# Retention ahead of two MLPs: the batches' chunks alternate, and scores and state use four quarters of the array

## The chip, the core and the metric

The kernel runs on one core of a Trainium2 chip. Its engines work side by side, each through its own instructions in order: PE (TensorE, with PEld for its weight loads), ACT (ScalarE), DVE (VectorE), POOL (GpSimd) and SP (SyncE), which issues nearly all transfers. They wait for one another by semaphores. The metric is the time of one execution on the device, in microseconds.

## The reference

```python
# q, k, v: batch 2, 8 heads, 576 positions, 64 features
scores = scale * np.matmul(q, k.transpose(0, 1, 3, 2))
Dmat = np.where(rel >= 0, gamma[:, None, None] ** rel[None, :, :], 0.0)   # rel = i - j
attn = np.matmul(scores * Dmat, v)
x = attn.transpose(0, 2, 1, 3).reshape(B * S, H * D)                      # 1152 x 512
for e in range(4):                                                        # F = 1024
    out += p[:, e:e + 1] * (np.maximum(x @ w1[e], 0.0) @ w2[e])
h = out @ w_in                                                            # 2048 wide
g = h * np.tanh(softplus(h))
return g @ w_out
```

## The kernel before

**Retention.** The sequence of a batch is cut into 9 chunks of 64 positions, 18 in all (`CHUNKS`). Inside a chunk the masked scores of 64 queries and 64 keys times v are taken; what comes from earlier chunks is a state, k transposed times v for each head. A decay factor for each key is put into v ahead (`v_decay`, POOL) and one for each query into the output (`decayed`, DVE), so the mask is of zeros and ones and the state is a plain sum, which stays in PSUM. A chunk is one transfer of 512 KB into one of six slots of `qkv`: partitions 0 to 63 (`KEYS`) hold v and k by positions, 64 to 127 (`FEATS`) hold k and q by features. An output is one matmul of 128 rows for each head: the masked scores (which replace k in `KEYS`, `masked` on DVE) and q (in `FEATS`) against v (`KEYS`) and the state, which ACT copies out of PSUM over k of the next chunk (`state_copy`). Batch 0's nine chunks come first, then batch 1's. All matmuls of the retention are fp32; each shows as two records in the trace.

**Turns.** 19 turns (`TURNS`) run on PE. Turn c has the scores of chunk c+1 and the state of chunk c, interleaved by heads (`scores_and_state`, lines 448 and 452), then the output of chunk c-1 (`output`, line 488). Scores read rows 64 to 127 of the array and write 64 columns, state reads rows 0 to 63 and writes the other 64. Between them stand halves of tiles of layer one of expert 0 (`AFTER_SCORES`, `AFTER_OUTPUT`): a tile is 128 of the 1024 hidden features for the first 384 tokens (`plain_products`), four inner blocks of three fp32r matmuls (`three`, lines 494 to 496: high by high, high by low, low by high), and needs the first six chunks' x. Eight tiles fit in turns 7 to 18. `keep_warm` runs matmuls on zeros (line 626): 9 ahead of chunk 0, 5 behind its scores, 3 in turn 0 and 8 in turn 6.

**The other engines in a turn.** DVE: `masked`, `decayed` of the chunk before, at times `rows` (a table of decay), `plain_lo` (the low half of a relu tile, line 849), `first_lo` (the low half of x, line 843). ACT: `state_copy` (line 696), `plain_hi` (relu and high half, line 713), `first_hi` (line 702), `job_hi` for weights (line 368; sums: line 364). POOL: `v_decay` two chunks ahead (line 1025), `job_lo` (line 395; a job of kind "s" makes four sums of weight blocks, lines 382 to 387, and their low half, line 390). `IN_TURN` says which weight jobs stand in which turn, one for each; the eight raw slots of weights (`RAW`) come free as jobs finish.

**Behind the turns** PE runs layer two of the first four tiles (`second(0, q)`, q = 0 to 11, three for each of w2's first four units), then stages of seven products by sums of blocks (`product`; the first that needs sums of x is P6) with layer two of the stage before between them, for four experts and the last MLP. DVE and ACT make the sums of x once the last chunk is through.

**Transfers.** SP loads chunk 0, the table of decays and mask, then chunks 1 to 5, then by turns a weight unit (256 KB) and a chunk, from weight 0 behind the landing of chunk 3. ACT loads the probabilities and the rest of the table.

## Time and profile before

| what | value |
|---|---|
| median of 3 runs | 626.67 us (625.93 to 629.63) |
| profiled execution, first to last instruction | 625.2 us |
| PE busy | 618.1 us (99%) |
| DVE, ACT, POOL busy | 271.6, 237.0, 285.0 us (43%, 38%, 46%) |
| chain that ended last | PE 97% |
| granted clock of TensorE | 1.00 |
| loaded from HBM | 47.45 MB, 80 GB/s over the span |

Busy is the share of the span in which an engine had an instruction running. PE's share counts pipelined matmuls and the filler on zeros alike. In the timelines each line gives the start in us from the first instruction, the time taken, the engine, the line of the kernel, the operation, what it writes and reads, its shape and the count where like ones were merged; in brackets the idle time of the engine ahead of it and what ended it. "issue" is an end that the profile does not show.

### The profile page before, as it was taken

To read this page: it belongs to the slowest core of one execution; us is meant where nothing else is said; L and a number is where in the kernel's file an instruction comes from. 1 tells how busy PE (TensorE), PEld (TensorE's weight loads), DVE (VectorE), ACT (ScalarE), POOL (GpSimd) and SP (SyncE) were. 2 spreads that over 40 slices of the span, in tenths; PEclk is the share of its full clock that TensorE was granted. 3 is DMA by queue.
4 is the path that set the end of the run, shared out by engine and by line. 5 is a ranking of instruction groups with operands and counts; after the bars stand their busy time and mean duration, and the time that the engine had idled before them with its cause. 6 is when DMAs were issued, how large, how long until landed. Compare 5 with 4: busy or idle time off the path is not lost.

```text
span 625.2 us, 9507 instructions
## 1 busy us (share of the span) xinstructions
PE 618.1 (99%) x3773; PEld 553.7 (89%) x3773; DVE 271.6 (43%) x388; ACT 237.0 (38%) x459; POOL 285.0 (46%) x239
## 2 busy tenths in 40 slices
PE   8999999999999999999999999999999999999997
PEld 5788899999999999999999899988989999989996
DVE  5646854433154433154433154434545432324334
ACT  3446423432223432123442223435455454334431
POOL 4657645553435542535543635532435553443300
PEclk9999999999999999999999999999999999999999
DMA  8955312332102321212312212321211233201002
GB/s 271 318 185 174 106 48 68 101 89 63 51 35 68 102 79 57 68 35 67 102 67 69 69 35 67 88 81 35 68 34 35 68 117 85 68 0 52 1 0 102
DMA packets 25147, 50.43 MB, mean 81 GB/s; under 512 B 2896, under 2 KB 3216, under 8 KB 25104
## 3 DMA queue, kind: packets, MB, share of 16 engines
q1 hardware_dynamic: 24816, 49.66, 25.4%
q8 instruction: 31, 0.51, 0.3%
q10 hardware_dynamic: 288, 0.17, 0.1%
q14 instruction: 12, 0.10, 0.0%
HBM read 47.45 MB, written 2.36 MB: 80 GB/s over the span
## 4 chain that ended last, share of the span: by engine, by line
PE 97%; DMA 1%; DVE 1%; issue 0%; ACT 0%; SPq 0%; DVEq 0%; ACTq 0%
PE bank L494 31%; PE bank L496 30%; PE bank L495 30%; PE bank L448 2%; PE bank L488 2%; DMA qkv<-in_chunks 1%; PE bank L619 1%; PE bank L452 1%; PE bank L626 0%; DVE acc_sb L895 0%; DVE acc_sb L899 0%; ACT qkv L696 0%; DVE qkv L822 0%; DVE h_lo L856 0%; SPq L418 0%
## 5 line engine op out<-in xcount | busy, mean ns | idle before, releaser
L395 POOL TENSOR_TENSOR w_lo<-w_raw,w_hi 128x512 fp32r<-128x512 f32 x96 | 132.2, 1389 | 150.7 <-ACT w_hi L368 148.9
L494 PE MATMUL bank<-w_hi,h_hi 128*128 128x512 f32 x432 | 168.8, 391 | 0.0
L496 PE MATMUL bank<-w_hi,h_lo 128*128 128x512 f32 x432 | 168.4, 390 | 0.0
L495 PE MATMUL bank<-w_lo,h_hi 128*128 128x512 f32 x432 | 168.3, 390 | 0.0
L882 DVE TENSOR_TENSOR h_act<-part,bank 128x384 f32<-128x384 f32 x96 | 52.9, 552 | 169.7 <-PE bank L496 168.9
L390 POOL TENSOR_TENSOR ws<-ws_f,ws 128x1024 fp32r<-128x1024 f32 x24 | 57.6, 2400 | 145.1 <-ACT ws L364 145.1
L496 PEld LDWEIGHTS bank<-w_hi,h_lo 128*128 128x128 f32 x432 | 81.1, 188 | 16.9
L495 PEld LDWEIGHTS bank<-w_lo,h_hi 128*128 128x128 f32 x432 | 81.1, 188 | 12.3
L494 PEld LDWEIGHTS bank<-w_hi,h_hi 128*128 128x128 f32 x432 | 81.0, 188 | 12.2
L732 ACT ACTIVATE part<-bank 128x384 f32<-128x384 f32 x72 | 35.4, 491 | 139.3 <-PE bank L496 139.3
L849 DVE SCALAR_TENSOR_TENSOR h_lo<-h_act,h_hi 128x384 fp32r<-128x384 f32 x64 | 74.3, 1170 | 20.6 <-ACT h_hi L722 20.0
L494 PE MATMUL bank<-xa_hi,w_hi 128*128 128x384 f32 x192 | 66.4, 346 | 0.0
L496 PE MATMUL bank<-xa_hi,w_lo 128*128 128x384 f32 x192 | 64.5, 336 | 0.0
L495 PE MATMUL bank<-xa_lo,w_hi 128*128 128x384 f32 x192 | 64.4, 336 | 0.0
L856 DVE TENSOR_TENSOR h_lo<-h_act,h_hi 128x384 fp32r<-128x384 f32 x48 | 38.2, 797 | 55.5 <-ACT h_hi L727 55.1
L368 ACT ACTIVATE w_hi<-w_raw 128x512 fp32r<-128x512 f32 x96 | 57.2, 618 | 0.0
L722 ACT ACTIVATE h_hi<-h_act 128x384 fp32r<-128x384 f32 x64 | 33.5, 525 | 58.5 <-DVE h_act L882 58.5
L495 PE MATMUL bank<-xt,ws 128*128 128x384 f32 x144 | 48.4, 336 | 0.0
L496 PE MATMUL bank<-xt,ws 128*128 128x384 f32 x144 | 48.4, 336 | 0.0
L494 PE MATMUL bank<-xt,ws 128*128 128x384 f32 x144 | 48.4, 336 | 0.0
L849 DVE SCALAR_TENSOR_TENSOR h_lo<-bank,h_hi 128x384 fp32r<-128x384 f32 x32 | 17.7, 554 | 59.9 <-ACT h_hi L713 59.9
L713 ACT ACTIVATE h_hi<-bank 128x384 fp32r<-128x384 f32 x32 | 15.7, 491 | 73.7 <-PE bank L496 73.7
(87 smaller groups left out, 911.4 us busy)
## 6 DMA issues: line engine op xcount, KB each, us to landing
w_raw<-in_weights SPq DMA_DIRECT2D x144, 256.0 KB, 2.8
qkv<-in_chunks SPq DMA_DIRECT2D x18, 512.0 KB, 4.6
out<-acc_sb SPq DMA_DIRECT2D x6, 256.0 KB, 2.0
out<-acc_sb SPq DMA_DIRECT2D x1, 768.0 KB, 3.6
consts<-in_consts ACTq DMA_DIRECT2D x1, 146.0 KB, 3.6
ident<-in_consts SPq DMA_DIRECT2D x1, 64.0 KB, 4.0
consts<-in_consts SPq DMA_DIRECT2D x1, 34.0 KB, 3.9
p_nat<-in_probs ACTq DMA_DIRECT2D x1, 18.0 KB, 3.6
```

The costliest lines, as they stand in the source:

```text
L368: act.activation(w_hi[int(kind == "w2")][:, x], w_raw[:, r % RAW], ACT.Copy).then_inc(s_wh, 1)
L390: pool.tensor_tensor(w_sum(x)[:, 1], ws_f[:, :], w_sum(x)[:, 0].bitcast(F32), ALU.subtract)\
L395: pool.tensor_tensor(w_lo[layer][:, x], w_raw[:, r % RAW], w_hi[layer][:, x].bitcast(F32), ALU.subtract).then_inc(s_wl, 1)
L494: pe.matmul(out, w[0], x[0], start=first, stop=False, **more)
L495: pe.matmul(out, w[0], x[1], start=False, stop=False, **more)
L496: return pe.matmul(out, w[1], x[0], start=False, stop=last, **more)
L713: act.activation(h_hi[:, tile_slot(s, i)], banks[6 + i % 2][:, 0:TC], ACT.Relu).then_inc(s_hh, 1)
L722: act.activation(h_hi[:, tile_slot(s, i)], h_act[:, i % 2], ACT.Relu).then_inc(s_hh, 1)
L732: act.activation(part[:, i], banks[6][:, 0:TC], ACT.Copy).then_inc(s_pt, 1)
L849: dve.scalar_tensor_tensor(h_lo[:, slot], full, 0.0, h_hi[:, slot].bitcast(F32), ALU.max, ALU.subtract).then_inc(s_hl, 1)
L856: dve.tensor_tensor(h_lo[:, slot], h_act[:, i % 2], h_hi[:, slot].bitcast(F32), ALU.subtract)\
L882: dve.tensor_tensor(h_act[:, i % 2], part[:, kept], banks[bank][:, 0:TC], op).then_inc(s_cc, 1)
```

## The change

- The chunks of the two batches alternate: chunk c is number c // 2 of batch c % 2 (`place`, `batch`). Each batch has a PSUM bank for its state. Tokens come out in this order, and the host puts them back.
- Decayed values go to a ring of four tiles `sv` (rows `KEYS`); the state for chunk c+2 is copied into its `FEATS` rows. v and k in the slot are no longer overwritten by them. POOL and ACT wait for the output that last read the place of the ring.
- Heads with even and odd number write the scores to the lower and the upper 64 partitions, likewise the state: scores of two heads and state of two heads follow each other on the four quarters of the array. The mask is two instructions of DVE, one for each half of the partitions.
- Outputs of the first six chunks alternate between banks 6 and 3.
- Tiles stand whole behind the output, in turns 7, 8, 10, 11, 13, 14, 16, 17. Relu and its low half stand first in the next turn on ACT and DVE. `first_lo` is one turn later, but for chunk 5. Weight jobs are moved (`JOBS_IN`): w2's first three units stand earlier, the sum job in turn 17, w2's units 3 to 5 in turn 18.
- The table and chunk 0 are one transfer on SP. Weights start behind the landing of chunk 6, ahead of chunk 8, one unit with each chunk.
- The filler is 7 and 3 matmuls; none in the turns.

```diff
...
+SLOT = 2 * HEADS * CH
+RING = 4
+def batch(c):
+    return c % BATCH
+def place(c):
+    return c // BATCH
 def has_state(c):
-    return c % PER_BATCH < PER_BATCH - 1
+    return place(c) < PER_BATCH - 1
...
-AFTER_SCORES = {8: (0, 1), 9: (1, 1), 10: (2, 1), 11: (3, 1), 12: (4, 1), 13: (5, 0), 14: (5, 1),
-                15: (6, 0), 16: (6, 1), 17: (7, 0), 18: (7, 1)}
-AFTER_OUTPUT = {7: (0, 0), 8: (1, 0), 9: (2, 0), 10: (3, 0), 11: (4, 0)}
-HIDDEN_IN = {t: c for c, (t, half) in AFTER_SCORES.items() if half}
-ROWS_IN = {0: 4, 1: 5, 6: 6, 7: 7, 8: 8}
-WARM_IN = {0: 3, 6: 8}
+TILE_IN = {7: 0, 8: 1, 10: 2, 11: 3, 13: 4, 14: 5, 16: 6, 17: 7}
+JOBS_IN = {6: (("w1", 0, 0),), 7: (("w1", 0, 1),), 8: (("w1", 0, 2),), 9: (("w1", 0, 3),), 10: (("w2", 0, 0),),
+           11: (("w1", 0, 4),), 12: (("w1", 0, 5),), 13: (("w2", 0, 1),), 14: (("w1", 0, 6),), 15: (("w1", 0, 7),),
+           16: (("w2", 0, 2),), 17: (("s", 0, 0),), 18: (("w2", 0, 3), ("w2", 0, 4), ("w2", 0, 5))}
+ROWS_IN = {5: 4, 9: 5, 11: 6, 13: 7, 15: 8}
+WARM_START, WARM_NEXT = 7, 3
...
+        sv = sb("sv", [P, RING, HEADS, DH])
...
-        ps_o = banks[3][:, 0:PAIRS * CH].rearrange("p (h c) -> p h c", h=PAIRS)
+        by_pairs = [bank[:, 0:PAIRS * CH].rearrange("p (h c) -> p h c", h=PAIRS) for bank in banks]
+        ps_s, ps_state = by_pairs[0:SCORES], by_pairs[4:4 + BATCH]
...
+        def ps_o(c):
+            return by_pairs[6 if c < PER_BLOCK and c % 2 == 0 else 3]
+        def score_rows(x):
+            return (KEYS, FEATS)[x]
+        def state_rows(x):
+            return (FEATS, KEYS)[x]
...
-            load_chunk(0)
-            sp.dma_start(consts[KEYS, 0:ROW0], consts_in[KEYS, 0:ROW0]).then_inc(s_const, 16)
+            sp.dma_start(loaded[:, lead - CONSTS:lead + SLOT], first_in).then_inc(s_slot[0], 16)
             load_chunk(1)
-            for c in range(2, 6):
-                if c > 2:
-                    chunk_there(c - 3)
-                load_chunk(c)
-            for u in range(UNITS):
-                chunk_there(3 + u)
-                load_weights(u)
-                chunk_there(4 + u)
-                load_chunk(6 + u)
-            for c in range(6 + UNITS, CHUNKS):
+            load_chunk(2)
+            for c in range(3, 8):
                 chunk_there(c - 3)
                 load_chunk(c)
-                load_weights(UNITS + c - 6 - UNITS)
-            sp.dma_start(ident[:, :], consts_in[:, CONSTS:]).then_inc(s_id, 16)
-            for r in range(UNITS + CHUNKS - 6 - UNITS, len(LOADS)):
+            for c in range(8, CHUNKS):
+                chunk_there(c - 2)
+                load_weights(c - 8)
+                load_chunk(c)
+            sp.dma_start(ident[:, :], ident_in).then_inc(s_id, 16)
+            for r in range(CHUNKS - 8, len(LOADS)):
                 load_weights(r)
...
-                return pe.matmul(ps_s[c % SCORES][:, h], by_feats(c, 0)[:, h], by_feats(c, 1)[:, h],
+                return pe.matmul(ps_s[c % SCORES][score_rows(h % 2), h // 2], by_feats(c, 0)[:, h], by_feats(c, 1)[:, h],
                                  start=True, stop=True)
             def state_head(c, h):
-                return pe.matmul(ps_state[h // HS][:, h % HS], by_keys(c, 1)[:, h], by_keys(c, 0)[:, h],
-                                 start=(c % PER_BATCH == 0 and h % HS == 0), stop=True, skip_group_check=True)
+                return pe.matmul(ps_state[batch(c)][state_rows(h % 2), h // 2], by_keys(c, 1)[:, h], sv[KEYS, c % RING, h],
+                                 start=(place(c) == 0 and h < 2), stop=True, skip_group_check=True)
...
-                        pe.wait_ge(s_sm, n - SCORES + 1)
+                        pe.wait_ge(s_sm, 2 * (n - SCORES + 1))
                 if has_state(c):
                     pe.wait_ge(s_vd, c + 1)
-                for h in range(HEADS):
-                    if has_state(c) and c > 0 and h % HS == 0:
-                        pe.wait_ge(s_st, 2 * states(c - 1) - 1 + h // HS)
+                    if place(c) > 0:
+                        pe.wait_ge(s_st, 2 * states(c - BATCH))
+                for hp in range(PAIRS):
                     if n < CHUNKS:
-                        mm = scores_head(n, h)
-                        if h == HEADS - 1:
+                        for x in range(2):
+                            mm = scores_head(n, 2 * hp + x)
+                        if hp == PAIRS - 1:
                             mm.then_inc(s_sc, 1)
                     if has_state(c):
-                        mm = state_head(c, h)
-                        if h == HEADS - 1:
+                        for x in range(2):
+                            mm = state_head(c, 2 * hp + x)
+                        if hp == PAIRS - 1:
                             mm.then_inc(s_kv, 1)
             def output(c):
                 pe.wait_ge(s_vd, c + 1)
-                pe.wait_ge(s_sm, c + 1)
+                pe.wait_ge(s_sm, 2 * (c + 1))
                 rows = KEYS
-                if c % PER_BATCH > 0:
+                if place(c) > 0:
                     rows = slice(0, P)
-                    pe.wait_ge(s_st, 2 * states(c - 1))
-                if c > 0:
+                    pe.wait_ge(s_st, 2 * states(c - BATCH))
+                if c >= PER_BLOCK:
                     pe.wait_ge(s_xt, c)
+                elif c > 1:
+                    pe.wait_ge(s_xt, c - 1)
                 for hp in range(PAIRS):
                     for x in range(2):
-                        mm = pe.matmul(ps_o[DH * x:DH * (x + 1), hp], qkv[rows, c % SLOTS, 0, 2 * hp + x],
+                        mm = pe.matmul(ps_o(c)[DH * x:DH * (x + 1), hp], sv[rows, c % RING, 2 * hp + x],
                                        qkv[rows, c % SLOTS, 1, 2 * hp + x], start=True, stop=True)
                 mm.then_inc(s_o, 1)
...
-            keep_warm(WARM)
+            keep_warm(WARM_START)
             pe.wait_ge(s_slot[0], landed(0))
             for h in range(HEADS):
                 mm = scores_head(0, h)
             mm.then_inc(s_sc, 1)
-            keep_warm(5)
+            keep_warm(WARM_NEXT)
             for c in range(TURNS):
                 if c < CHUNKS:
                     scores_and_state(c)
-                if c in AFTER_SCORES:
-                    plain_half(*AFTER_SCORES[c])
-                keep_warm(WARM_IN.get(c, 0))
                 if c > 0:
                     output(c - 1)
-                if c in AFTER_OUTPUT:
-                    plain_half(*AFTER_OUTPUT[c])
+                if c in TILE_IN:
+                    s, i = divmod(TILE_IN[c], ITEMS)
+                    plain_ready(s, i)
+                    plain_products(s, i, range(KT))
...
             def state_copy(c):
-                act.wait_ge(s_sc, c + 2)
                 act.wait_ge(s_kv, states(c))
-                for i in range(2):
-                    at = by_feats(c + 1, 0)[:, HS * i:HS * (i + 1)]
-                    act.activation(at, ps_state[i], ACT.Copy).then_inc(s_st, 1)
+                if c >= BATCH:
+                    act.wait_ge(s_o, c - BATCH + 1)
+                for x in range(2):
+                    act.activation(sv[FEATS, (c + BATCH) % RING, x::2], ps_state[batch(c)][state_rows(x)],
+                                   ACT.Copy).then_inc(s_st, 1)
...
             for c in range(TURNS):
+                if c - 1 in TILE_IN:
+                    plain_hi(*divmod(TILE_IN[c - 1], ITEMS))
                 if c < CHUNKS and has_state(c):
                     state_copy(c)
-                for t, at in HIDDEN_IN.items():
-                    if at == c:
-                        plain_hi(t // ITEMS, t % ITEMS)
...
-                dve.tensor_tensor(by_keys(c, 1), ps_s[c % SCORES], mask.unsqueeze(1).broadcast_to([CH, HEADS, CH]),
-                                  ALU.mult).then_inc(s_sm, 1)
+                for x in range(2):
+                    at = score_rows(x)
+                    dve.tensor_tensor(by_keys(c, 1)[:, x::2], ps_s[c % SCORES][at],
+                                      mask[at].unsqueeze(1).broadcast_to([CH, PAIRS, CH]), ALU.mult).then_inc(s_sm, 1)
...
             for c in range(TURNS):
+                if c - 1 in TILE_IN:
+                    plain_lo(*divmod(TILE_IN[c - 1], ITEMS))
                 if c < CHUNKS:
                     masked(c)
+                if c > 1 and c != PER_BLOCK + 1:
+                    first_lo(c - 2)
                 if c > 0:
                     decayed(c - 1)
                 if c in ROWS_IN:
                     rows(ROWS_IN[c])
-                for t, at in HIDDEN_IN.items():
-                    if at == c:
-                        plain_lo(t // ITEMS, t % ITEMS)
-                if c > 0:
+                if c == PER_BLOCK:
                     first_lo(c - 1)
+            first_lo(CHUNKS - 1)
...
             def v_decay(c):
                 pool.wait_ge(s_slot[c % SLOTS], landed(c))
-                v = by_keys(c, 0)
-                pool.tensor_tensor(v, v, key_decay[KEYS, c % PER_BATCH].unsqueeze(2).broadcast_to([CH, HEADS, DH]),
+                if c >= RING:
+                    pool.wait_ge(s_o, c - RING + 1)
+                pool.tensor_tensor(sv[KEYS, c % RING], by_keys(c, 0),
+                                   key_decay[KEYS, place(c)].unsqueeze(2).broadcast_to([CH, HEADS, DH]),
                                    ALU.mult).then_inc(s_vd, 1)
...
-                    pool.wait_ge(s_xl, c)
+                    if c > 1:
+                        pool.wait_ge(s_xl, c - 1)
                     job_lo(pool, job)
...
+        "first": np.concatenate([tables(), chunks[0].reshape(P, SLOT)], axis=1),
+        "chunks": chunks[1:],
+        "ident": np.eye(P, dtype=np.float32),
+        "probs": moe_domain_probs.reshape(BATCH, PER_BATCH, CH, MOE_EXPERTS).transpose(0, 2, 1, 3).reshape(P, -1),
         "weights": np.concatenate(weights),
...
-    nc = bacc.Bacc("TRN2", target_bir_lowering=False, num_devices=1)
+    nc = bacc.Bacc("TRN2", target_bir_lowering=False, num_devices=1, dynamic_dma_scratch_size=1024)
...
+    rows = run(nc, [{f"in_{n}": a for n, a in arrays.items()}], core_ids=[0]).results[0]["out"]
+    return np.ascontiguousarray(rows.reshape(PER_BATCH, BATCH, CH, DM).transpose(1, 0, 2, 3).reshape(TOKENS, DM))
```

## Rows read from the trace of the kernel before

**Rows 1.** Busy time by stretch: us, engine busy (instructions), clock, DMA share, GB/s.

```profile
0.00:62.20 62.20, 58.49 (x954) 46.59 (x954) 35.44 (x71) 29.32 (x72) 37.59 (x39) 1.00 0.71 238
62.20:625.20 563.00, 559.59 (x2824) 507.07 (x2820) 236.16 (x318) 207.69 (x389) 247.44 (x201) 1.00 0.21 63
```

**Rows 2.** Timeline of PE: start us, us, engine, line, operation, out<-in.

```profile
1.31 3.64 PE L626 MATMUL bank<-zeros 128*128 128x512 bf16 x9 [1.31 <-POOL zeros L1019]
5.95 1.25 PE L626 MATMUL bank<-zeros 128*128 128x512 bf16 x5
...
31.22 0.27 PE L448 MATMUL bank<-qkv 64*64 64x64 f32 x1
32.30 0.45 PE L494 MATMUL bank<-xa_hi,w_hi 128*128 128x384 f32 x1
...
33.54 0.69 PE L488 MATMUL bank<-qkv 128*64 128x64 f32 x16
34.16 0.44 PE L494 MATMUL bank<-xa_hi,w_hi 128*128 128x384 f32 x1
...
70.50 0.34 PE L494 MATMUL bank<-xb_hi,w_hi 128*128 128x384 f32 x1
...
72.61 0.39 PE L494 MATMUL bank<-w_hi,h_hi 128*128 128x512 f32 x1
```

**Rows 3.** Timeline of PE around 10.5 us, one line a record.

```profile
10.49 0.22 PE L448 MATMUL bank<-qkv 64*64 64x64 f32 x1
10.49 0.22 PE L488 MATMUL bank<-qkv 64*64 64x64 f32 x1
10.50 0.22 PE L452 MATMUL bank<-qkv 64*64 64x64 f32 x1
10.55 0.22 PE L452 MATMUL bank<-qkv 64*64 64x64 f32 x1
```

**Rows 4.** Busy time by stretch, the first 20 us.

```profile
0.00:12.00 12.00, 9.91 (x132) 5.91 (x134) 5.02 (x12) 2.62 (x6) 4.88 (x9) 1.00 0.80 266
12.00:16.00 4.00, 3.50 (x94) 2.97 (x89) 3.37 (x7) 2.10 (x6) 2.14 (x2) 1.00 0.91 291
16.00:20.00 4.00, 3.95 (x111) 3.59 (x113) 2.92 (x7) 2.22 (x7) 2.35 (x2) 1.00 0.94 329
```

**Rows 5.** Timeline of POOL, values of chunk 5 decayed as it landed.

```profile
13.55 1.03 POOL L1025 TENSOR_TENSOR qkv<-qkv,consts 64x512 f32<-64x512 f32 x1 [0.39 <-DMA qkv<-in_chunks]
```

**Rows 6.** Groups by line, 26 to 62 us: count, busy us, mean ns, idle before.

```profile
L843 DVE TENSOR_TENSOR xb_lo<-xf,xb_hi 128x256 fp32r<-128x256 f32 x6 | 3.4, 562 | 0.1
L837 DVE TENSOR_TENSOR xf<-bank,row_decay 128x256 f32<-128x256 f32 x10 | 4.2, 421 | 8.4 <-PE bank L488 8.4
L849 DVE SCALAR_TENSOR_TENSOR h_lo<-bank,h_hi 128x384 fp32r<-128x384 f32 x7 | 3.8, 547 | 0.0
...
L713 ACT ACTIVATE h_hi<-bank 128x384 fp32r<-128x384 f32 x7 | 3.4, 490 | 4.7 <-PE bank L496 4.7
L364 ACT ACTIVATE ws<-ws_f 128x1024 fp32r<-128x1024 f32 x1 | 1.1, 1058 | 0.5 <-POOL ws_f L387 0.5
...
L395 POOL TENSOR_TENSOR w_lo<-w_raw,w_hi 128x512 fp32r<-128x512 f32 x10 | 12.9, 1289 | 11.3 <-ACT w_hi L368 9.5 <-DVE xb_lo L843 1.8
L390 POOL TENSOR_TENSOR ws<-ws_f,ws 128x1024 fp32r<-128x1024 f32 x1 | 2.4, 2392 | 1.2 <-ACT ws L364 1.2
L382 POOL TENSOR_TENSOR ws_f<-w_raw 128x256 f32<-128x256 f32 x1 | 0.7, 747 | 0.2 <-DVE xb_lo L843 0.2
```

**Rows 7.** Line 843, x's low half: shortest, median and longest ns.

```profile
L843 DVE TENSOR_TENSOR xb_lo<-xf,xb_hi x12: 382/452/1931, 27.3 to 64.4; 128x256 fp32r<-128x256 f32 x6, 128x128 fp32r<-128x128 f32 x6
```

**Rows 8.** Timelines of PE and DVE behind 62.2 us.

```profile
62.20 0.50 PE L494 MATMUL bank<-w_hi,h_hi 128*128 128x512 f32 x1
...
74.64 0.34 PE L494 MATMUL bank<-xt,ws 128*128 128x384 f32 x1
...
70.85 0.96 DVE L925 TENSOR_TENSOR xt<-xs_a,xt 128x768 fp32r<-128x768 f32 x1
```

More of the change, by code:

```diff
@@ L135, in add @@
         JOBS.append(job)
-    for u in range(UNITS):
-        add(IN_TURN, 5 + u, "w1", 0, u)
-    for u in range(3):
-        add(IN_TURN, 12 + u, "w2", 0, u)
-    add(IN_TURN, 15, "s", 0, 0)
-    for u in range(3, 6):
-        add(IN_TURN, 13 + u, "w2", 0, u)
+    for turn, jobs in JOBS_IN.items():
+        for job in jobs:
+            add(IN_TURN, turn, *job)
     add(IN_STAGE, 1, "w2", 0, 6)
@@ L240, in build @@
         x2_c = acc_sb[:, TT:2 * TT].rearrange("p t d -> p (t d)").rearrange("p (k c) -> p k c", k=KT)
+        qkv = loaded[:, lead:].rearrange("p (s w h c) -> p s w h c", s=SLOTS, w=2, h=HEADS)
+        consts = loaded[:, lead - CONSTS:lead]
         key_decay = consts[:, 0:MASK0].rearrange("p (c h) -> p c h", h=HEADS)
[L243 removed]
+        mask = consts[:, MASK0:ROW0]
         row0 = consts[:, ROW0:STEP0].rearrange("p (h c) -> p h c", h=PAIRS)
@@ L247, in build @@
         banks = [ctx.enter_context(nc.psum_tensor(f"bank{i}", [P, 512], F32)) for i in range(8)]
-        ps_s = [banks[i][KEYS, :].rearrange("p (h c) -> p h c", h=HEADS) for i in range(SCORES)]
-        ps_state = [banks[i][FEATS, 0:HS * DH].rearrange("p (h c) -> p h c", h=HS) for i in range(2)]
-        ps_o = banks[3][:, 0:PAIRS * CH].rearrange("p (h c) -> p h c", h=PAIRS)
+        by_pairs = [bank[:, 0:PAIRS * CH].rearrange("p (h c) -> p h c", h=PAIRS) for bank in banks]
+        ps_s, ps_state = by_pairs[0:SCORES], by_pairs[4:4 + BATCH]
         s_slot = [sem(f"s_slot{i}") for i in range(SLOTS)]
-        s_const = sem("s_const")
-        s_rows = sem("s_rows")
         s_id = sem("s_id")
@@ L522, in plain_products @@
                     mm.then_inc(s_l1, 1)
-            def plain_half(t, half):
-                s, i = divmod(t, ITEMS)
-                if half == 0:
-                    plain_ready(s, i)
-                plain_products(s, i, range(2 * half, 2 * half + 2))
             def product(s, j):
@@ L830, in decayed @@
             def decayed(c):
-                i = c % PER_BATCH
+                i = place(c)
                 if i > 0:
@@ L1047, in tables @@
     c = np.arange(PER_BATCH, dtype=np.float64)
-    consts = np.zeros((P, CONSTS + P))
+    consts = np.zeros((P, CONSTS))
     keys = gamma[None, None, :] ** (MID - CH * c[None, :, None] - i[:, None, None])
     consts[KEYS, 0:MASK0] = keys.reshape(CH, MASK0)
-    consts[KEYS, MASK0:ROW0] = i[:, None] <= i[None, :]
+    consts[:, MASK0:ROW0] = np.tile(i[:, None] <= i[None, :], (2, 1))
     rows = gamma[:, None] ** (i[None, :] - MID) / np.sqrt(DH)
@@ L1088 @@
     build(nc, *args, out)
-    return run(nc, [{f"in_{n}": a for n, a in arrays.items()}], core_ids=[0]).results[0]["out"]
+    rows = run(nc, [{f"in_{n}": a for n, a in arrays.items()}], core_ids=[0]).results[0]["out"]
+    return np.ascontiguousarray(rows.reshape(PER_BATCH, BATCH, CH, DM).transpose(1, 0, 2, 3).reshape(TOKENS, DM))
```

33 lines of the change are left out of this document (12 added, 21 removed).

## The prediction

> **What bounds the kernel now.** I read the busy time by stretch first. TensorE (PE) is busy 559.6 of the 563.0 us behind 62.2 us, where the first matmul of layer two starts, and 58.5 of the 62.2 us ahead of it [rows 1]. The change leaves the work behind 62.2 us as it is (DVE, ACT and POOL are under half busy there), so its worth is how much earlier that matmul starts, minus what comes late behind it. Call its start T; T is 62.2 us now. PE hardly waits ahead of T either, but 25 matmuls of that stretch are filler on a tile of zeros (9, 5, 3 and 8 by the code), and they hide waiting.
>
> Next the timeline of PE, which gives prices from the start of one block to the start of the next [rows 2]. Scores with state: 31.22 to 32.30, 1.08 us. A half tile of layer one: 1.24 us (32.30 to 33.54). An output: 33.54 to 34.16, 0.61 us.
>
> **The four quarters.** Before, the scores use one quarter of the array and the state another: two streams of 16 records in 1.08 us. An output uses both column halves, 16 records in two streams of 8, and takes 0.61 us. With scores and state each over both column halves, 32 records run in four streams of 8, so I price the block as an output, 0.61 us, 0.47 us less. No row shows four streams. Three are there at 10.49 us: scores, output and state start within 0.01 us, and the state again at 10.55 [rows 3], 0.05 to 0.06 us later, as it does beside one other stream (1.08 us for 16 records, with 0.14 for filling and draining). The bounds are 0.61 and 1.08 us; I take 0.61, since the third stream cost nothing.
>
> The Trainium skill speaks against this: "TensorE: Matmul & The Clock Gate", section "Wait — 56ns, not 53.3ns?", says that start to start never falls below about 25 ns, however small the matmul. By that, 32 records would take 0.80 us, and an estimate by that page is a block of about 0.95 us, a saving of 0.13. The trace has starts closer than that, on different quarters, so I do not follow it.
>
> **Whole tiles.** 12 matmuls, 70.50 to 72.61 us, take 2.11 us, or 0.176 each [rows 2]. A whole tile is a half (1.24) and six more (1.04), 2.28 us, where two halves took 2.48. The change of array shape is paid once, and eight tiles save 1.6 us.
>
> **When the first tile can start.** Up to turn 7 the chunks bind. Weights no longer go ahead of chunk 8. Chunk 8 is there once 0.02 (probabilities) + 0.74 (tables and chunk 0) + 8 x 0.524 + 0.26 (the first weights) = 5.2 MB have come. The windows give 3.2 MB by 12 us, 4.4 by 16 and 5.7 by 20 [rows 4]. Chunk 5, at 3.3 MB by the same count, landed just ahead of 13.55 us [rows 5], when about 3.6 MB had come: what is in flight behind adds 0.3 to 0.4 MB. So chunk 8 lands at 5.6 MB, about 19.6 us (bounds 18.6 and 20.6: 0.3 MB more or less in flight). In turn 6 POOL decays chunk 8's values (1.03 us [rows 5]) before it makes the first weights' low half (1.29 [rows 6]), and tile 0 waits for that: 19.6 + 0.1 + 1.0 + 1.3 = 22.0 us. From turn 8 a chunk and weights, 0.79 MB, need 2.4 us, less than the 3.5 us of a turn with a tile and 2.7 on the mean of a group of three, so transfers bind no more.
>
> **From there to T, by PE alone.** 8 tiles x 2.28 = 18.2; 9 blocks of scores and state (turns 8 to 16) x 0.61 = 5.5; 11 outputs x 0.61 = 6.7. Together 30.4, so T = 52.4 us.
>
> **What is late next.** In a turn ACT now first makes the relu of the tile of the turn before, then copies state, then the high half of x, then weights; DVE makes the tile's low half, two masks, x's low half of two turns back, then the decayed output. From chunk 6 on, output c waits for the decayed output c-1. The turns behind 8, 11 and 14 have no tile, and PE runs ahead of that chain there. From the start of tile 1, PE is ready for output 9 after 2.28 + 3 x 0.61 = 4.11 us. The chain that releases it is the tile (2.40, with its drain), relu on ACT 0.49, low half 0.50, two masks 0.68, x's low half 0.36, decayed output 0.41: 4.84 us. The two masks of 64 x 256 are priced by the decayed output, which reads 256 columns of PSUM too: 0.42 each [rows 6], of which 0.08 lies under the next; x's low half is its fastest, 0.38 to 0.42, less a like overlap [rows 7]. The difference, 0.73 us, falls three times (outputs 9, 12, 15), together 2.1 us. Behind the waiting output stand tiles 2, 4 and 6, so T moves by all of it: 54.5 us.
>
> DVE's work between tiles of SBUF is slower at times: x's low half took from 0.38 to 1.93 us [rows 7], 0.56 on the mean for 128 x 256 [rows 6], and I take POOL's instructions for what holds it up. Turns are shorter now and POOL's work is the same, so I add 0.5 us to each of the three stalls, 1.5 in all (bounds 0 and 3.9, the latter where each waits for a whole POOL instruction, 1.3). T = 56.0 us.
>
> **What is late behind T.** The weight sums of job s are now in turn 17 (turn 15 before), and w2's fourth unit behind it. From T backward, tile 6 starts at T - 5.8; ACT, DVE and x's low half end 4.3 us later, at T - 1.5, and release POOL. Then four sums (4 x 0.74), the high half on ACT (1.06), the low half 2.39, the unit's low half 1.29 [rows 6]: T + 6.2. PE wants it at the tenth of twelve products, 9 x 0.69 = 6.2 us behind T (62.20 to 70.50 is 8.30 for twelve [rows 2, 8]). No margin is left. I put 0.8 us on it (bounds 0 and 1.9, with DVE's x sums between POOL's instructions). The x sums on DVE: the first low half is done at 71.8 now and wanted at 74.64 [rows 8], and DVE gets to them a little sooner relative to T, so nothing there.
>
> **At no cost.** One load in place of two and chunk 0: same bytes. Decayed values in a ring: same POOL instruction, other target. State copies: same two of ACT, now two turns ahead of use. Other host order: none. Fewer fillers: 15 gone, all ahead of tile 0, hidden behind chunk 8; without that cover they would only save.
>
> **Sum.** 62.2 - 56.0 - 0.8 = 5.4 us earlier, of 625.2: 619.8. The median shown is 626.7, 1.5 above the profiled execution, so 621.3.
>
> **Rivals.**
> A, the loop of ACT and DVE keeps up: no hindrance by POOL, no wait for w2. T = 54.5 us, gain 7.7; with chunk 8 up to a us earlier, 8.2. For it: DVE is busy 35.4 of the 62.2 us ahead of T [rows 1]. Against: the slow ones of today [rows 7]. 619.0, or 618.5. 0.32.
> B, the quarters do not overlap beyond two. The block stays at 1.08 us, nine of them cost 4.2 us more, but the three stalls (3.6 us) vanish since PE no longer runs ahead; T is 52.4 + 4.2 = 56.6, with w2's 0.8 a gain of 4.8: 621.9. For it: no row has four streams. Against: [rows 3]. 0.14. The Trainium skill's limit of 25 ns (page and section above) would land between B and my sum.
> C, the gain is given back behind T: POOL and DVE, with the same work in less time, hold w2's unit and the x sums by 2 to 4 us more. 623 to 625.5. Against: 2.8 us of margin on the x sums [rows 8]. 0.08.
> D, slower: the clock. The first nine fillers took 3.64 us, 0.40 each, the next five 1.25, 0.25 [rows 2]: PE began at half its clock (1.2 GHz) and rose to 2.4 though the page grants 1.00 all through. Seven fillers, then a wait, then 1.2 us of work per 1.6 us chunk may not lift it. At half clock a turn is 2.4 us and a tile 4.4. Every two us at half clock costs one; to be slower than before, the low level must last from tile 0 (22.0 us) for more than 11 us, to about turn 10. It would give 627 to 634, the latter if it lasts for 25 us. Against: PE is dense from tile 0, as it was here when it rose. 0.05.
>
> **Chances.** My sum 0.41 (its own range 619.5 to 622.5), A 0.32, B 0.14, C 0.08, D 0.05. About 1% (6.3 us) is what a measurement of this kernel can tell from no change: under 620.4 is faster. A but for 0.02, a quarter of my sum and 0.02 of B lie there, 0.42; slower by over 1% (from 633) is half of D, 0.03; the remainder, 0.55, is within. The range reaches over A and B and most of C: 617.5 (chunk 8 at 18.6 us and A, with half a us over) to 625.0.
>
> **What would show it.** Sixteen score and sixteen state records within 0.7 us: right for the quarters; 1.1 us: B. Tile 0 at 22.0 us. PE idle about a us ahead of outputs 9, 12 and 15, put down to DVE's decayed output. T at 56.0. A gap of PE some 6 us behind T, put down to w2's low half on POOL. Filler or score records at twice their length past 10 us: D. Wrong would be the sum if chunk 8 lands off 19.6 by a us or more, which moves T by the like, or if ACT's queue delays the relu of each tile, which my chain counts as free.

## The result, and the profile after

| | before | after |
|---|---|---|
| median | 626.81 us (625.93 to 629.63, 4 runs) | 633.48 us (631.61 to 635.27, 4 runs) |
| ratio to before, 95% interval | | 1.0104 (1.0079 to 1.0129) |
| profiled execution | 625.2 us | 633.4 us |
| T, the first matmul of layer two | 62.20 us | 66.62 us |
| from T to the end | 563.0 us | 566.8 us |
| granted clock, mean | 1.00 | 0.985 |

The change is slower by 1.0%, where 621.3 us (617.5 to 625.0) was predicted. Both halves of the program lost: T came 4.4 us later, not 6.2 earlier, and the work behind it takes 3.8 us more. The profiled execution is the slowest of the four, 1.8 us above their median and with the lowest mean clock, so what is read from it below adds up to more than the medians are apart.

From the page of the kernel after: busy time, the granted clock in 40 slices of 15.8 us, and the shares of the chain that ended last.

```profile
PE 611.6 (97%) x3758; PEld 550.4 (87%) x3758; DVE 281.9 (45%) x406; ACT 238.6 (38%) x459; POOL 288.4 (46%) x239
...
PEclk8798999999999999999999999999999999999999
...
PE 88%; DVE 8%; issue 2%; ACT 1%; DMA 1%; POOL 0%; DVEq 0%; POOLq 0%
```

PE was 97% of the chain before and is 88% now, and DVE has 8%. The granted clock, full all through before, is below full in the first slices. The busy time by stretch, cut at the new T, to be held against [rows 1]:

```profile
0.00:66.60 66.60, 51.42 (x938) 43.52 (x938) 42.63 (x88) 29.13 (x69) 34.76 (x36) 0.87 0.68 222
66.60:633.40 566.80, 560.21 (x2823) 506.90 (x2820) 239.27 (x318) 209.47 (x390) 253.66 (x204) 1.00 0.21 63
```

PE is busy 7 us less ahead of T, as the change wants, and idle 15 us there where it was idle 4. DVE is busy 42.6 us instead of 35.4.

**The quarters and the whole tile.** Timeline of PE in the kernel after: start us, us, engine, line (454 scores, 458 state, 498 output, 504 to 506 tile):

```profile
31.66 0.44 PE L504 MATMUL bank<-xa_hi,w_hi 128*128 128x384 f32 x1
...
33.94 0.27 PE L454 MATMUL bank<-loaded 64*64 64x64 f32 x2
33.96 0.27 PE L458 MATMUL bank<-sv,loaded 64*64 64x64 f32 x2
34.05 0.23 PE L454 MATMUL bank<-loaded 64*64 64x64 f32 x2
...
34.57 0.69 PE L498 MATMUL bank<-loaded,sv 128*64 128x64 f32 x16
35.18 0.27 PE L454 MATMUL bank<-loaded 64*64 64x64 f32 x2
```

The whole tile takes 2.28 us (31.66 to 33.94). The 32 records of scores and state take 0.63 us to the output's start; the output takes 0.61 more.

**The waits of PE ahead of T**, from the timeline of PE in the kernel after, the wait in brackets:

```profile
10.87 0.80 PE L498 MATMUL bank<-loaded,sv 64*64 64x64 f32 x10 [2.09 <-DVE loaded L826]
...
25.69 0.69 PE L504 MATMUL bank<-xa_hi,w_hi 128*128 128x384 f32 x1 [1.60 <-POOL w_lo L408]
...
37.18 0.69 PE L498 MATMUL bank<-loaded,sv 128*64 128x64 f32 x16 [1.30 <-DVE xf L841]
...
48.61 1.12 PE L498 MATMUL bank<-loaded,sv 128*64 128x64 f32 x16 [2.82 <-DVE xf L841]
...
59.70 0.69 PE L498 MATMUL bank<-loaded,sv 128*64 128x64 f32 x16 [1.34 <-DVE xf L841]
...
66.00 0.69 PE L498 MATMUL bank<-loaded,sv 128*64 128x64 f32 x16 [0.42 <-DVE xf L841]
```

Outputs 0, 9, 12, 15 and 17 and tile 0 stand here; a wait of 1.25 us ahead of output 6 (23.41) comes shortly before tile 0. Tile 0 starts at 25.69 us. The waits at 37.18, 48.61 and 59.70 are those of outputs 9, 12 and 15. The output at 48.61 takes 1.12 us, not 0.69.

The wait of tile 0 is put down to POOL, but it goes back to DVE. Values of chunk 8 are decayed at 21.49, as it lands; POOL is free for the first weights' low half at 22.5 us, and that starts at 24.38. The timelines of POOL and of ACT (705 x's high half, 381 weights) there:

```profile
21.49 1.03 POOL L1031 TENSOR_TENSOR sv<-loaded 64x512 f32<-64x512 f32 x1 [1.83 <-DMA loaded<-in_chunks]
24.38 1.26 POOL L408 TENSOR_TENSOR w_lo<-w_raw,w_hi 128x512 fp32r<-128x512 f32 x1 [1.85 <-ACT w_hi L381]
```

```profile
23.30 0.42 ACT L705 ACTIVATE xa_hi<-x_tmp 128x256 fp32r<-128x256 f32 x1 [1.13 <-DVE x_tmp L841]
23.62 0.61 ACT L381 ACTIVATE w_hi<-w_raw 128x512 fp32r<-128x512 f32 x1
```

ACT makes the high half of the weights only behind that of x, which had waited for a decayed output of DVE.

**The clock.** Busy time by stretch of the kernel after (the number behind the five engines is the granted clock):

```profile
10.00:15.00 5.00, 4.13 (x106) 4.05 (x108) 3.93 (x8) 1.17 (x3) 3.11 (x3) 0.58 0.71 247
15.00:25.00 10.00, 6.71 (x204) 5.68 (x200) 9.05 (x23) 6.34 (x16) 3.74 (x4) 0.84 0.85 270
25.00:30.00 5.00, 4.31 (x17) 3.87 (x21) 0.41 (x1) 1.04 (x4) 3.89 (x4) 0.50 0.86 269
```

A granted clock of 0.50 is 1.2 of 2.4 GHz. It was at 0.50 from about 10.8 to 17.5, 24.5 to 31.2 and 48.3 to 51.7 us. Tile 0 at 25.69 lasted 4.14 us, 1.86 more than a tile at full clock.

**Behind T.** The timeline of DVE in the kernel after, three of x's eight sums (lines 964 to 969 and 929):

```profile
68.69 0.95 DVE L964 TENSOR_TENSOR xs_a<-xf 128x768 f32<-128x768 f32 x1
...
70.42 3.15 DVE L967 TENSOR_TENSOR xs_a<-xf,xs_a 128x768 f32<-128x768 f32 x1
...
81.35 2.05 DVE L929 TENSOR_TENSOR xt<-xs_b,xt 128x768 fp32r<-128x768 f32 x1
```

The timeline of POOL in the same stretch, the end of a job's weight sums and then the low halves of five units:

```profile
69.67 3.09 POOL L403 TENSOR_TENSOR ws<-ws_f,ws 128x1024 fp32r<-128x1024 f32 x1 [1.24 <-ACT ws L377]
72.72 9.86 POOL L408 TENSOR_TENSOR w_lo<-w_raw,w_hi 128x512 fp32r<-128x512 f32 x5
```

And the timeline of PE, at w2's fourth unit:

```profile
74.75 0.50 PE L504 MATMUL bank<-w_hi,h_hi 128*128 128x512 f32 x1 [1.71 <-POOL w_lo L408]
```

The eight sums took 14.7 us (68.7 to 83.4), where they took 9.5 before; the fifth started at 70.85 in [rows 8] and starts at 75.55 now. A second wait of PE, 1.2 us at 84.85, is for a copy of ACT (line 735). ACT reaches it only behind the high half of a relu, which waited for DVE's addition at 83.32, and that stood behind the sums.

### The profile page after: what moved, and what is told of

Its sections match the earlier page's. It is cut to its first block, busy times and chain, and to the rows that moved or that the text cites. A ratio compares the mean times of both kernels' runs of the same rounds, so it can differ in the third digit from the quotient of the medians.

```text
span 633.4 us, 9497 instructions
## 1 busy us (share of the span) xinstructions
PE 611.6 (97%) x3758; PEld 550.4 (87%) x3758; DVE 281.9 (45%) x406; ACT 238.6 (38%) x459; POOL 288.4 (46%) x239
## 4 chain that ended last, share of the span: by engine, by line
PE 88%; DVE 8%; issue 2%; ACT 1%; DMA 1%; POOL 0%; DVEq 0%; POOLq 0%
PE bank L504 29%; PE bank L506 29%; PE bank L505 29%; DVE loaded L826 1%; DVE xt L929 1%; DVE xb_lo L847 1%; DMA p_nat<-in_probs 1%; PE bank L622 1%; DVE xf L841 1%; DVE xs_a L967 0%; ACT h_hi L716 0%; ACT w_hi L381 0%; PE bank L498 0%; DVE xa_lo L847 0%; DVE x_tmp L841 0%
## 5 line engine op out<-in xcount | busy, mean ns | idle before, releaser
L408 POOL TENSOR_TENSOR w_lo<-w_raw,w_hi 128x512 fp32r<-128x512 f32 x96 | 134.3, 1412 | 151.6 <-ACT w_hi L381 151.6
L505 PEld LDWEIGHTS bank<-w_lo,h_hi 128*128 128x128 f32 x432 | 81.1, 188 | 12.2
L735 ACT ACTIVATE part<-bank 128x384 f32<-128x384 f32 x72 | 35.4, 491 | 139.5 <-PE bank L506 139.5
```

Source lines behind the costliest of these rows:

```text
L408: pool.tensor_tensor(w_lo[layer][:, x], w_raw[:, r % RAW], w_hi[layer][:, x].bitcast(F32), ALU.subtract).then_inc(s_wl, 1)
L505: pe.matmul(out, w[0], x[1], start=False, stop=False, **more)
L735: act.activation(part[:, i], banks[6][:, 0:TC], ACT.Copy).then_inc(s_pt, 1)
```

## The experiments

The start of tile 0, T, the rest behind it and the time of x's sums come from each profiled execution, in us. Ratios are against the kernel before, on the same chip, with 95% intervals.

| kernel | tile 0 | T | rest | sums | median us | ratio |
|---|---|---|---|---|---|---|
| before | 25.79 | 62.20 | 563.0 | 9.5 | 626.8 | 1 |
| after | 25.69 | 66.62 | 566.8 | 14.7 | 633.5 | 1.0104 (1.0079 to 1.0129) |
| e1 filler in turns | 26.74 | 64.96 | 566.8 | 14.7 | 632.8 | 1.0107 (1.0084 to 1.0129) |
| e2 probabilities late | 24.09 | 64.39 | 569.8 | 14.7 | 636.1 | 1.0161 (1.0140 to 1.0182) |
| e3 decayed first | 24.90 | 60.24 | 567.0 | 15.2 | 629.4 | 1.0048 (1.0020 to 1.0077) |
| e4 two quarters | 25.48 | 61.91 | 566.5 | 14.7 | 630.0 | 1.0064 (1.0046 to 1.0081) |
| e5 e3, w2 early | 23.15 | 58.43 | 566.4 | 14.7 | 628.5 | 1.0016 (0.9995 to 1.0036) |
| e6 e3, two quarters | 26.23 | 60.98 | 566.7 | 14.7 | 628.6 | 1.0026 (1.0007 to 1.0046) |
| e7 mended | 24.66 | 58.40 | 569.2 | 14.7 | 627.2 | 0.9998 (0.9978 to 1.0017) |
| e8 e7, two quarters | 24.82 | 62.51 | 567.7 | 14.2 | 632.1 | 1.0077 (1.0055 to 1.0099) |
| e9 e7, POOL waits | 22.97 | 56.74 | 563.5 | 12.0 | 622.7 | 0.9926 (0.9907 to 0.9944) |
| e10 after, POOL waits | 24.36 | 63.14 | 565.1 | 12.5 | 630.5 | 1.0048 (1.0029 to 1.0067) |
| e11 e9, no filler in turns | 25.69 | 61.78 | 563.4 | 12.0 | 624.4 | 0.9961 (0.9944 to 0.9979) |
| e12 e9, probabilities first | 24.11 | 57.86 | 563.4 | 12.0 | 622.8 | 0.9929 (0.9906 to 0.9952) |

A single T is good to some us only: it depends on where the clock falls in that execution. After and e10 do the same up to T, and theirs are 3.5 us apart. The medians and ratios decide. Where the two differ, the ratios weigh more, since each is taken against the kernel before on the same chip.

### e1: filler that keeps the clock up

```diff
-WARM_START, WARM_NEXT = 7, 3
+WARM_START, WARM_NEXT = 9, 5
+WARM_IN = {1: 9, 6: 3, 7: 5, 10: 5, 13: 12, 16: 6}   # matmuls on zeros, ahead of a turn's output
+WARM_TILE = {7: 7}                                   # and ahead of its tile
```

> The changed kernel with matmuls on zeros where its PE waited: 9 and 5 at the start, 9 ahead of output 0, 3 ahead of output 5, 5 ahead of output 6, 7 ahead of tile 0, and 5, 12 and 6 ahead of outputs 9, 12 and 15. The changed kernel takes 633.5 us, the one before 626.8. Clock theory (PE fell to half its clock in three stretches, 10.9 to 17, 25.5 to 31 and 48 to 52 us, and that is the loss): full clock in all of them, tile 0 in 2.3 us in place of 4.1, layer two of the first tiles (66.6 us now) at 61 to 62, and 628 to 629 us. Chain theory (DVE with ACT and POOL sets the pace of the turns, and PE's clock only fills its waits): the records are short again but the waits ahead of outputs 9, 12 and 15 grow by as much, at least 631.5 us.

The clock stayed at 1.00, in its busy time by stretch:

```profile
10.00:26.70 16.70, 13.40 (x356) 9.61 (x352) 13.46 (x30) 9.50 (x25) 7.70 (x8) 1.00 0.76 274
26.70:65.00 38.30, 36.06 (x567) 29.65 (x568) 26.21 (x52) 18.08 (x44) 23.12 (x21) 1.00 0.62 202
```

The median is only 0.7 us below the kernel after, and the ratios cannot be told apart, as the chain theory had it. So lifting the clock does not bring the time back. From tile 0 to T it took 38.2 us for 40.9, but tile 0 came 1.1 us later, behind filler of its own (T came 1.7 us earlier, no more); e1 does not part the filler's price from the clock's.

### e2: the probabilities behind x's sums

The wait for the probabilities and the four instructions on them (lines 931 to 940) stand behind x's sums on DVE.

> The changed kernel, but DVE's four instructions on the probabilities (5.7 to 8.0 us) stand behind the sums of x, at 85 us. Chain theory: the decay tables start 2 us sooner, the first mask at about 8 us in place of 9.9, tile 0 at about 23.5 in place of 25.7, and 631 us. Clock theory: the 2.1 us wait of PE ahead of output 0 is gone, so the first fall of the clock with it: records of the scores of chunks 2 to 6 are short, and the later two falls stay: 630 to 631 us. Both say faster; if it is the same 633, neither the start of DVE nor the first fall counts.

Both theories had said faster. Tile 0 came 1.6 us sooner, but the ratio rose by 0.6%. Behind T the rest grew by 3.0 us: the second wait of PE became 2.6 us, since DVE's addition now stands behind the four instructions too, and the clock then fell (0.72 granted from 84 to 90 us). What was moved off one chain had been put onto another.

### e3: the decayed output ahead of x's low half

```diff
-                if c > 1 and c != PER_BLOCK + 1:
-                    first_lo(c - 2)
                 if c: decayed(c - 1)        # in short; it first waits for the low half two chunks back, in chunks 2 to 5
+                if c > 1 and c != PER_BLOCK + 1:
+                    first_lo(c - 2)
```

> The changed kernel, but in each turn DVE makes the decayed output ahead of the low half of x of two turns back. Chain theory: the output of the next turn, and behind it the tile, wait for the decayed output, and the low half (0.4 us alone, up to 1.6 beside POOL) no longer stands ahead of it: each of the waits ahead of outputs 9, 12 and 15 (1.3, 2.8, 1.4 us) shrinks by 0.4 to 1.2 us, 630 to 631 us. Clock theory: the wait of 2.8 us falls under what brings the clock down, the third fall goes too, 629 us. If the waits are set by ACT's relu instead, nothing changes: 633.5.

Two instructions of DVE change places and 4.1 us of the median are back (3.5 by the ratios), the largest effect of one edit to the kernel after by the medians; by the ratios e10 gives as much. The kernel after shows why. The timeline of its DVE ahead of output 12 (line 853 low half of a tile's relu, 826 masks, 847 x's low half, 841 decayed output):

```profile
42.94 0.94 DVE L847 TENSOR_TENSOR xb_lo<-xf,xb_hi 128x256 fp32r<-128x256 f32 x1
43.91 0.42 DVE L841 TENSOR_TENSOR xf<-bank,row_decay 128x256 f32<-128x256 f32 x1
...
45.71 0.56 DVE L853 SCALAR_TENSOR_TENSOR h_lo<-bank,h_hi 128x384 fp32r<-128x384 f32 x1 [1.05 <-ACT h_hi L716]
46.19 0.86 DVE L826 TENSOR_TENSOR loaded<-bank,loaded 64x256 f32<-64x256 f32 x2
47.08 0.93 DVE L847 TENSOR_TENSOR xb_lo<-xf,xb_hi 128x256 fp32r<-128x256 f32 x1
48.04 0.42 DVE L841 TENSOR_TENSOR xf<-bank,row_decay 128x256 f32<-128x256 f32 x1
```

The timeline of its ACT (705 x's high half, 381 weights, 716 relu):

```profile
44.37 0.42 ACT L705 ACTIVATE xb_hi<-xf 128x256 fp32r<-128x256 f32 x1 [2.02 <-DVE xf L841]
44.69 0.61 ACT L381 ACTIVATE w_hi<-w_raw 128x512 fp32r<-128x512 f32 x1
45.21 0.47 ACT L716 ACTIVATE h_hi<-bank 128x384 fp32r<-128x384 f32 x1
```

It is a ring. The tile's last matmul ended at 43.68, but its relu started at 45.21, behind x's high half and a weight unit on ACT, which had waited for the decayed output of 43.91; and that stood behind x's low half. The late relu makes the next masks, x's low half and decayed output late, and output 12 waits 2.8 us. With the decayed output first, outputs 9 and 12 wait the same short time, and output 15 still 1.54 us (timeline of PE of e3):

```profile
34.91 0.69 PE L498 MATMUL bank<-loaded,sv 128*64 128x64 f32 x16 [0.64 <-DVE xf L843]
...
43.91 0.69 PE L498 MATMUL bank<-loaded,sv 128*64 128x64 f32 x16 [0.64 <-DVE xf L843]
...
53.80 0.69 PE L498 MATMUL bank<-loaded,sv 128*64 128x64 f32 x16 [1.54 <-DVE xf L843]
```

### e4, e6 and e8: two quarters and one mask

The layout of before is put back for scores and state: one quarter each, one mask of 64 x 512 in place of two of 64 x 256. In e4 it is the only edit to the kernel after, in e6 it stands on e3, in e8 on e7.

```diff
-                return pe.matmul(ps_s[c % SCORES][score_rows(h % 2), h // 2], ...
+                return pe.matmul(ps_s[c % SCORES][KEYS, h], ...
-                for x in range(2): dve.tensor_tensor(by_keys(c, 1)[:, x::2], ...   # in short
+                dve.tensor_tensor(by_keys(c, 1), ...
```

> The changed kernel with scores on one quarter and state on one other, as before the change, and one mask of 64 x 512 in place of two of 64 x 256; ring, order of batches, whole tiles and transfers stay. Chain theory: the block of scores and state goes from 0.6 back to 1.08 us, but DVE gets 0.26 us back in each of 18 turns (0.86 for two masks, 0.60 for one); PE had waits to fill, so 630 to 632 us. Clock theory: PE is busier in turns 0 to 6, and the first fall may go: 629 to 631. If the four quarters paid on PE, it is slower by up to 17 x 0.47 = 8 us less the waits: 635 to 637.

> e3_decayed_first with scores and state on two quarters and one mask, as e4_two_quarters. Chain theory: with both remedies (decayed output sooner, 0.26 us of DVE back in each turn) no wait for DVE is left ahead of outputs 9, 12 and 15, the clock stays up, and PE alone sets layer two's start: 25.0 for tile 0 + 8 x 2.28 + 9 x 1.08 + 11 x 0.61 = 59.7 us, near e3's 60.2; 628 to 629 us. If the quarters pay as soon as DVE allows, it is slower than e3 (629.4) by up to 4 us; if the mask's split still costs, faster, 627 to 628.

> e7_mended with scores and state on two quarters and one mask. It tells what the four quarters are worth once the order of DVE and POOL is mended. Chain theory: nine blocks of 1.08 us for 0.61 are 4.2 us of PE, of which the waits left in e7 (1 to 2.5 us) and DVE's 0.26 us a turn give back most: within 1.5 us of e7 to either side. If the chain no longer binds in e7, it is 3 to 4 us slower than e7.

The sign turns with what binds. Taking the quarters away gained 3.5 us in the kernel after (2.5 by the ratios), 0.8 on e3 (1.4 by the ratios; the intervals overlap), and cost 4.9 us on e7. The reason for the gain is DVE. Its groups by line and shape, 0 to 67 us in the kernel after:

```profile
L826 DVE TENSOR_TENSOR loaded<-bank,loaded 64x256 f32<-64x256 f32 x36 | 15.0, 417 | 1.2 <-PE bank L458 0.5
```

Behind one mask of 64 x 512 the next instruction starts after 0.60 us, behind a pair of 64 x 256 after 0.89 (46.19 to 47.08 above): 0.29 us more in every turn, ahead of the decayed output that PE waits for. The reason for the loss is PE. Busy time by stretch of e7, from tile 0 to T:

```profile
24.60:58.40 33.80, 33.65 (x557) 28.29 (x557) 26.27 (x56) 19.52 (x46) 24.37 (x23) 1.00 0.72 246
```

The same stretch of e8:

```profile
24.80:62.50 37.70, 37.68 (x556) 32.37 (x556) 22.42 (x45) 18.91 (x46) 24.32 (x22) 1.00 0.70 227
```

In both PE has hardly any idle time left (0.15 and 0.02 us, with the same filler), and the second needs 3.9 us more: the blocks of turns 8 to 16, nine at 0.63 and at 1.08 us. So the quarters are worth 4 us on PE, and the kernel after never got them. What the alternating batches and the whole tiles are worth was not tried by taking them back alone.

### e5 and e7: the other mends

e5 is e3 with w2's fourth unit in turn 16 instead of 18. e7 is e5 with the probabilities in turn 7 and filler placed by e5's waits.

```diff
-           16: (("w2", 0, 2),), 17: (("s", 0, 0),), 18: (("w2", 0, 3), ("w2", 0, 4), ("w2", 0, 5))}
+           16: (("w2", 0, 2), ("w2", 0, 3)), 17: (("s", 0, 0),), 18: (("w2", 0, 4), ("w2", 0, 5))}
...
+WARM_START, WARM_NEXT = 9, 5
+WARM_IN = {1: 8, 10: 3, 13: 3, 16: 6}    # and 4 behind output 5, 1 ahead of tile 0
```

> e3_decayed_first (629.4 us) with w2's fourth unit one place ahead of the weight sums (turn 16), so that POOL has its low half before layer two of the first tiles wants it. Layer two starts at 60.2 us there and 62.2 in the kernel before, yet the rest takes 567.1 us against 563.0. Theory of POOL's order: 1.8 us of that is PE's wait for that unit, and goes: 627.6 us. The other 2 us or more come from the sums of x on DVE, 0.9 us alone and 1.9 to 3.1 beside POOL's low halves, and stay or shrink by one low half's time: 626.5 to 627.6. Rival, the sums alone: PE waits as long, only later, since DVE's sums end at the same time: 629.

> e5_w2_early with DVE's instructions on the probabilities in turn 7, where it waits for tile 0 (not ahead of the turns), and matmuls on zeros: 9 and 5 at the start, 8 ahead of output 0, 4 behind output 5, 1 ahead of tile 0, and 3, 3 and 6 ahead of outputs 9, 12 and 15. Chain theory: the turns start 1.6 us sooner (e2_probs_late had tile 0 at 24.1 for 25.7 us), and 1 us at most from the clock, since records at full clock mostly lengthen PE's waits: layer two at 58 us and 624.5 to 625.5 us, better than the kernel before. Clock theory: tile 0 takes 2.3 us for 4.0 and nothing of that is lost: layer two at 56.5 and 623.5.

T was 58.4 us in both (in e5 by an earlier tile 0, which its edit does not touch), but the rest did not fall: the wait for w2's unit (1.8 us in e3) is gone and another stands in its place, 2.8 us at 76.2 for ACT's copy behind the late sums, as e5's rival had it. Both medians came out above the forecasts. Busy time by stretch around this wait in e5:

```profile
72.00:78.00 6.00, 3.25 (x17) 2.64 (x16) 3.89 (x4) 1.32 (x4) 5.01 (x5) 1.00 0.21 75
78.00:84.00 6.00, 6.00 (x32) 5.42 (x31) 4.25 (x5) 2.61 (x5) 4.75 (x4) 1.00 0.19 65
```

And in e7:

```profile
72.00:78.00 6.00, 3.21 (x13) 2.61 (x11) 3.89 (x4) 0.90 (x2) 5.00 (x5) 0.79 0.26 76
78.00:84.00 6.00, 6.00 (x22) 5.41 (x22) 1.76 (x2) 1.96 (x3) 3.79 (x3) 0.64 0.06 11
```

The same wait, once with the clock full behind it and once at half for nearly 7 us; e7's rest is 2.8 us longer. That is this execution, the slowest of e7's ten; in four of them the mean clock was 1.00. By the medians e7 is 1.3 us faster than e5.

### e9 and e10: POOL waits for x's sums

```diff
             # POOL, ahead of the jobs behind the turns
+            pool.wait_ge(s_tl, 4)          # DVE's four low halves of x's sums are there
```

> e7_mended (627.2 us), but POOL waits for DVE's last low half of the x sums before it makes the low halves of w2's last two units and the next weight sums. In e5 and e7 the eight instructions on the x sums took from 60.1 to 74.7 us, 0.9 to 3.2 us each, beside POOL's; in the kernel before 64.9 to 74.4 in all. ACT's copy of the third product stands behind the relu that waits for DVE, and PE waits 2.8 us for it at 76.2 us. Theory of the shared hindrance: the last four (1.5 to 2.0 us each) go to about 1 us, DVE is free 3 us sooner, PE's wait goes, and with it the fall of the clock behind it in e7: 622.5 to 624, faster than the kernel before (626.5). Rival: the sums are slow of themselves, or POOL's later start makes w2's units or the next weight sums late: 627 or more.

> The changed kernel (633.5 us) with nothing but that wait of POOL. Behind the start of layer two it takes 566.8 us where the kernel before takes 563.0; 1.7 us is PE's wait for w2's fourth unit, which this does not touch, and 1.2 us the wait at 84.85 us behind the x sums. Theory of the shared hindrance: 632.3 us, the first wait left as it is. Rival: as e9_pool_waits, no gain or a loss, 633.5 or more.

One wait for POOL, and behind T no wait of PE over 0.2 us is left. The timeline of DVE in e9 (the last sums are line 940 in this kernel):

```profile
65.85 1.94 DVE L940 TENSOR_TENSOR xt<-xs_a,xt 128x768 fp32r<-128x768 f32 x1
67.71 0.95 DVE L940 TENSOR_TENSOR xt<-xs_b,xt 128x768 fp32r<-128x768 f32 x1
```

The timeline of its POOL (line 410 is w_lo):

```profile
62.98 3.99 POOL L410 TENSOR_TENSOR w_lo<-w_raw,w_hi 128x512 fp32r<-128x512 f32 x2
70.47 2.85 POOL L410 TENSOR_TENSOR w_lo<-w_raw,w_hi 128x512 fp32r<-128x512 f32 x2 [3.51 <-DVE xt L940]
```

While POOL rests (66.97 to 70.47), a sum takes 0.95 us. The rest is 563.5 us, as before, and e9 is faster than the kernel before by 0.7%: the change with its chains mended beats both kernels. The mends were not tried on the kernel before. On the kernel after alone the wait gives 3.0 us (e10, 3.5 by the ratios), more than the 1.2 expected; 1.7 of it is in the rest, and the remainder lies ahead of T, where the two kernels do the same, and is not explained.

### e11 and e12: what of e9 matters

e11 is e9 with the kernel after's filler (7 and 3, none in the turns). e12 is e9 with the probabilities first again.

> e9_pool_waits (622.7 us) with the filler of the changed kernel, 7 and 3 matmuls on zeros and none in the turns. It prices the clock once the chain of DVE, ACT and POOL is mended. Clock theory: PE still waits about 2 us ahead of output 0 and around turn 7, falls to half its clock there, and tile 0 (and what stands beside it) costs 1.5 to 2 us more, which now nothing hides: 624.5. Chain theory: the waits left take it, as in e1_filler, where the filler gave 0.7 us: 623 to 623.5.

> e9_pool_waits with DVE's instructions on the probabilities ahead of the decay tables again, as in the changed kernel. It prices the late start of DVE: the probabilities land at 5.7 us there (4.4 in the kernel before), and the first mask ended 1.7 us later than it could. Chain theory: tile 0 starts 1.5 us later and with it all behind: 624. Rival: chunks and their landing set tile 0, and DVE catches up by then: 622.7 to 623.

e12 equals e9: no worth of the place of the probabilities shows. e11 is 1.7 us slower (2.2 by the ratios, whose intervals just touch) and spreads more (622.4 to 627.0, e9's runs 621.9 to 623.7); its profile, the slowest of its ten, has the granted clock at 0.92 from tile 0 to T and T at 61.8. So the filler, of which nothing showed in the kernel after (e1), brings about 2 us once DVE no longer holds PE up.

## Why the prediction was wrong, step by step

Three steps failed: tile 0's start was put down to the chunks alone, each relu was taken to start with its tile's end, and x's sums behind T were put at nothing. The waits that came of it brought the clock down, which the sum had at full.

The predicted execution was 619.8 us and the profiled one 633.4, 13.6 apart (the medians 12.2): tile 0 3.7, waits ahead of T 2.5, the low clock from tile 0 on about 4.4 (what is left of T; the starts of the blocks account for 3.9 of it), behind T 3.0.

**Four quarters: right.** 0.61 was taken, 0.63 came; rival B is out. The records of scores and state start 0.01 to 0.02 us apart, each group of four some 0.06 us behind the last. The Trainium skill's limit of 25 ns from start to start ("TensorE: Matmul & The Clock Gate", section "Wait — 56ns, not 53.3ns?") does not hold across quarters in this trace. The term of it that the sum lacked is the price on DVE: the two masks were priced at 0.68 us from start to start and cost 0.89, and the turn's second mask stood in no comparison with the one that it replaced.

**Whole tiles: right.** 2.28 us taken, 2.28 measured, at full clock.

**Tile 0 at 22.0 us: wrong by 3.7.** The step that failed is "up to turn 7 the chunks bind". DVE was busy 9.05 of the 10 us from 15 to 25 us. Output 0 waited 2.1 us for the first masks, which DVE began at 9.86, behind the probabilities and three tables of decay. Loads 6 and 7 of the chunks need the slots that outputs 0 and 1 free, so chunk 8 landed at 21.4, not 19.6. And the chain from there to tile 0 had POOL alone in it: the first weights' low half waited 1.85 us for ACT's high half, which stood behind a decayed output of DVE. The two, 1.8 and 1.85 us, are the 3.7. Which instruction of DVE counts most here was not isolated: with the probabilities out of the way tile 0 started between 23.0 (e9) and 25.7 us (e11), with them between 23.2 (e5) and 26.7 (e1, with its filler).

**Three stalls of 0.73 us, and 0.5 for POOL: the place right, the size wrong.** They came ahead of outputs 9, 12 and 15, put down to the decayed output, with 1.3, 2.8 and 1.3 us; with small ones 6.1 in all, not 3.6 (three times 0.73 are 2.2, where the sum has 2.1). So rival A, that the loop keeps up, is out. The chain priced the relu as starting with the tile's end. That was named as what would make the sum wrong, and it did: ACT's queue held it for 1.5 us, because its work ahead waited for the decayed output. Where that output goes first (e3), two of the three waits are 0.64 us, near the 0.73 of the sum; the third is 1.54.

**The clock, rival D, given 0.05.** It happened, at 10.8 to 17.5, 24.5 to 31.2 and 48.3 to 51.7 us: late in or just behind waits of PE of 2.1 us and of 2.8 us, and at 24.5 behind two waits of 0.7 and 1.25 us and in one of 1.6, with little work between. D asked for 11 us at half clock behind tile 0 and got about 9. That the measured 633.5 lies in its 627 to 634 is luck: the clock is about 4.4 of the 13.6 us. The rival was judged alone, as if PE were dense from tile 0; but it was the other misses, the waits, that brought it on. What it cost on top of them stays open to some us: e1 removed it whole, at the price of its own filler, and gained 0.7 us.

**"The x sums ... nothing there": wrong by about 1.7 of the 3.0 us behind T.** That is what e10 gives back there; 0.9 is w2's unit, and 0.4 stays open. Rival C, given 0.08, foresaw this, 2 to 4 us more behind T than the sum had, and 3.0 came. The row of 0.96 us in [rows 8] was one of a moment in which POOL was idle; in the same profile the first two sums took 2.05 each. In the kernel after POOL works without a pause from 69.67 to 86.5 us, and each of the six sums from 70.42 on takes 1.9 us or more. The sum at 70.42 shows it: it began while POOL's instruction of 69.67 ran, until 72.76, and ended 0.8 us behind that. The Trainium skill ("SBUF — State Buffer", section "Who interferes with whom") says that an instruction of DVE with both inputs in SBUF contends with one of POOL that reads SBUF. The trace agrees on both sides: 0.95 us alone and up to 3.15 beside POOL with two inputs in SBUF, and 0.42 us for each decayed output and mask, which read PSUM, whatever POOL did. e9 shows the cause: POOL held back, the last three sums at 0.95 us and 563.5 us behind T.

**w2's fourth unit, 0.8 us: right in place, 1.7 in size.** But it was no margin to be bought alone: e5 removed it, and the wait for the sums took over.
